# A fused attention and two-expert kernel: the first three chunks in a prologue of their own with a native fp32 first expert, and the slots left over made up two a step

## What is computed

```python
for t in range(S):
    cur = einsum('bhd,bhe->bhde', u[None] * kt, vt)
    y[:, :, t] = einsum('bhd,bhde->bhe', rt, state + cur)
    state = wt[:, :, :, None] * state + einsum('bhd,bhe->bhde', kt, vt)
x = y as 3072 tokens x 384
h = x @ w_in                      # 384 -> 1024
solu = h * softmax(h)
ln = (solu - mean) / sqrt(var + 1e-6) * g_ln
x2 = ln @ w_out                   # 1024 -> 384
h2 = x2 @ w_in2                   # 384 -> 2048
out = maximum(0.01 * h2, h2) @ w_out2   # 2048 -> 384
```

## Time and profile before

| | us |
|---|---|
| median of 3 runs (lowest, highest) | 835.58 (833.29, 835.66) |
| the profiled execution | 836.03 |
| its span, first to last instruction | 834.3 |
| TensorE busy in it | 787.2 |
| DVE / ACT / POOL busy in it | 538.0 / 320.0 / 215.6 |
| mean granted TensorE clock | 0.971 of full |

### The profile page before, as it was taken

The page is one execution under the profiler, slowest core; times in us unless marked ns, Lnnn a source line. Parts: engine busy times, 40 slices in busy tenths (PEclk is TensorE's granted clock), DMA queues, the critical chain, the costliest instruction groups (busy, mean ns, idle before and its releaser), DMA issues.

```text
span 834.3 us, 11926 instructions
## 1 busy us (share of the span) xinstructions
PE 787.2 (94%) x4570; PEld 746.7 (89%) x4570; DVE 538.0 (64%) x1116; ACT 320.0 (38%) x604; POOL 215.6 (26%) x224
## 2 busy tenths in 40 slices
PE   2866799999999999999999999999999999999996
PEld 1644689999999999999999999999999999999996
DVE  7777866666765775666766776657766676543332
ACT  2335433434432443334433443443433333334332
POOL 4667732123132132123122132123122222100000
PEclk9976599999999999999999999999999999999999
DMA  7772112113012032023022032023022030000000
GB/s 195 225 242 57 33 26 57 26 32 86 22 36 58 1 86 58 5 54 86 1 58 57 1 86 57 1 57 85 1 57 57 2 86 29 1 1 29 1 1 31
DMA packets 18844, 43.47 MB, mean 52 GB/s; under 512 B 2272, under 2 KB 14688, under 8 KB 18400
## 3 DMA queue, kind: packets, MB, share of 16 engines
q1 hardware_dynamic: 14736, 33.24, 16.5%
q10 hardware_dynamic: 4048, 9.44, 3.3%
HBM read 37.95 MB, written 4.72 MB: 51 GB/s over the span
## 4 chain that ended last, share of the span: by engine, by line
PE 86%; DVE 2%; ACT 1%; issue 0%; DVEq 0%; ACTq 0%
PE BANKS L961 59%; PE MISC L961 23%; PE BANKS L1072 2%; PE MISC L991 1%; PE MISC L984 1%; DVE state L768 0%; DVE att L722 0%; DVE RL L866 0%; ACT RH L629 0%; DVE Rraw L860 0%; DVE A L742 0%; ACT Rraw L622 0%; ACT W4H L556 0%; DVE ke L730 0%; ACT EXP L561 0%
## 5 line engine op out<-in xcount | busy, mean ns | idle before, releaser
L622 ACT ACTIVATE Rraw<-BANKS 128x384 f32<-128x384 f32 x128 | 62.9, 491 | 244.3 <-PE BANKS L961 244.2
L860 DVE TENSOR_TENSOR Rraw<-BANKS,Rraw 128x384 f32<-128x384 f32 x128 | 71.3, 557 | 124.5 <-ACT Rraw L622 124.0
L961 PE MATMUL BANKS<-RH,W4H 128*128 128x384 f32 x384 | 138.5, 361 | 0.9 <-DVE RL L866 0.8
L961 PE MATMUL BANKS<-X2H,W3H 128*128 128x384 f32 x384 | 130.4, 340 | 0.2 <-DVE X2L L872 0.2
L961 PE MATMUL BANKS<-X2L,W3H 128*128 128x384 f32 x384 | 129.2, 336 | 0.0
L961 PE MATMUL BANKS<-RH,W4L 128*128 128x384 f32 x384 | 129.0, 336 | 0.0
L961 PE MATMUL BANKS<-RL,W4H 128*128 128x384 f32 x384 | 129.0, 336 | 0.0
L961 PE MATMUL BANKS<-X2H,W3L 128*128 128x384 f32 x384 | 129.0, 336 | 0.0
L442 POOL TENSOR_TENSOR A<-ke,att 112x512 f32<-112x512 f32 x21 | 31.4, 1494 | 256.7 <-DVE att L734 256.7
L629 ACT ACTIVATE RH<-Rraw 128x384 fp32r<-128x384 f32 x128 | 67.1, 524 | 79.3 <-DVE Rraw L860 79.3
L730 DVE RECIPROCAL ke<-att 112x128 f32<-112x128 f32 x96 | 90.1, 941 | 0.0
(11 more groups left out here) (119 smaller groups left out, 1562.1 us busy)
## 6 DMA issues: line engine op xcount, KB each, us to landing
att<-rkw SPq DMA_DIRECT2D x48, 288.0 KB, 4.8
rtok<-r_tok SPq DMA_DIRECT2D x24, 192.0 KB, 5.0
ktok<-k_tok SPq DMA_DIRECT2D x24, 192.0 KB, 5.0
vtok<-v_tok SPq DMA_DIRECT2D x24, 192.0 KB, 5.1
out<-OUT SPq DMA_DIRECT2D x8, 576.0 KB, 6.0
W3raw<-w_in ACTq DMA_DIRECT2D x1, 3072.0 KB, 11.5
W4raw<-w_out ACTq DMA_DIRECT2D x1, 3072.0 KB, 24.7
W1raw<-w_in ACTq DMA_DIRECT2D x1, 1536.0 KB, 9.3
```

The lines of the kernel that those rows point to most:

```text
L622: nc.scalar.activation(Rraw[:, fp % 2, :], PR[fp % 2][:, 0:ST], ACT.Copy, scale=0.01).then_inc(act_slope, 1)
L860: nc.vector.tensor_tensor(Rraw[:, fp % 2, :], PR[fp % 2][:, 0:ST], Rraw[:, fp % 2, :], ALU.max).then_inc(dve_relu, 1)
L961: return nc.tensor.matmul(dst, lhsT, rhs, start=start, stop=stop, skip_group_check=True)
```

## The change

All engines get a prologue written out by hand for chunks 0 to 2 in place of `item` over 28 slots and the 8 M1 steps. In it:

- scores of a chunk go to two whole banks, are masked two pairs at a time (`first_mask`), and A holds all four pairs. Chunk 0's queries and keys go in halves (`portions`);
- the first expert is a plain fp32 product of x and the loaded W1 (`first_expert`), and the second product of expert one is plain fp32 of W2 and LN transposed and scaled by the gain, chunk by chunk (`first_out`, ACT's `take_ln`);
- ACT's queue loads all four weights at the start in the order W1, W3, W2, W4. W3 is split in the prologue (low parts on POOL), W1 and W2's low parts are made on POOL in the first M2 stage, W4's on DVE there; pieces are 768 columns;
- 24 slots are done when the M2 stage begins. In its first twelve steps two slots a step are run, the second behind `cons`; from the thirteenth on it is one, as before.

In all batches: the gain is no longer in W2 but a scale operand of the M1 copies on ACT and DVE; reciprocals have a tile of their own (ki), the range check sums ki and ct in two ACT passes in place of one POOL sum and one ACT pass; the decayed state is made on POOL (`decayed_state`), and DVE updates the state by two instructions of 192 columns in place of one of 384 and four of 96. The decay scans of the first chunks take their floor from PSUM.

```diff
+if opening and fp <= STEPS:
+    done = [min(CPS * SLOTS + 2 * j, F1 + LEAD + j) for j in (f, f + 1)]
+else:
+    done = [fp + LEAD - 1, fp + LEAD]
...
+def scores_of(m, a):
+    if m == 1:
+        return BANKS[:, (KM - 1 + a // 2) * 512:(KM + a // 2) * 512]
+    if m == 2:
+        return BANKS[:, a // 2 * 512:(a // 2 + 1) * 512]
+    return MISC[:, (a // 2 + 1) * 512:(a // 2 + 2) * 512]
...
+GROUPS = (4, 4, 8, 8)
...
+    def decayed_state(b, m):
+        wait(pool, dve_state, states(b, m - 1))
+        last = ct[:, m % 2, :, CH - 1:CH].broadcast_to([PD, PAIRS, PC])
+        nc.gpsimd.tensor_tensor(fresh[:, :, :], state[:, :, :], last, ALU.mult).then_inc(pool_decay, 1)
...
+    def low_part(w, g):
+        pool.wait_ge(split_hi[w], g + 1)
+        if w == 0:
+            pool.wait_ge(pe_h, 2 * CPS)
+        if w == 1:
+            pool.wait_ge(pe_cons, F1)
+        nc.gpsimd.tensor_tensor(group(los[w], w, g), group(raws[w], w, g),
...
+            if opening(b, kind, so):
+                if f < GROUPS[0]:
+                    low_part(0, f)
+                if F1 <= f < F1 + GROUPS[1]:
+                    low_part(1, f - F1)
...
+    own_token(0, 0, 0)
+    decayed_queries(0, 1)
+    own_token(0, 0, 1)
+    end_keys(0, 1)
+    decayed_state(0, 1)
+    own_token(0, 1, 0)
+    decayed_queries(0, 2)
+    for g in range(2):
+        low_part(2, g)
+    own_token(0, 1, 1)
+    end_keys(0, 2)
+    row_scale(0, 0)
+    decayed_state(0, 2)
+    own_token(0, 2, 0)
+    for g in range(2, 4):
+        low_part(2, g)
+    own_token(0, 2, 1)
+    decayed_queries(0, 3)
+    row_scale(0, 1)
+    end_keys(0, 3)
+    for g in range(4, 6):
+        low_part(2, g)
+    row_scale(0, 2)
+    for g in range(6, 8):
+        low_part(2, g)
...
+    def take_range(b, m):
+        wait(act, dve_inv, chunks(b, m, PAIRS, PAIRS))
+        for i, part in enumerate((ki[:, :, :], ct[:, m % 2, :, :])):
+            wait(act, act_range, chunks(b, m, 2, i))
+            nc.scalar.activation(junk[:, :, :], part, ACT.Copy,
+                                 accum_out=spread[:, bass.ds(chunks(b, m, 2, i), 1)]).then_inc(act_range, 1)
...
+        if attend and s == 7 and exists(b, m) and exists(b, m + 1):
+            take_range(b, m + 1)
...
+    def take_ln(m):
+        wait(act, pe_m1, m)
+        for f in range(F1):
+            wait(act, pe_lnT, m * 2 + f // 4 + 1)
+            nc.scalar.activation(first_ln[:, f, :], PR[f // 4][:, f % 4 * CH:(f % 4 + 1) * CH], ACT.Identity,
+                                 scale=gain[:, f:f + 1]).then_inc(act_lnT, 1)
...
+                if f % 2 == 0 and f // 2 + 2 < GROUPS[3]:
+                    high_part(3, f // 2 + 2)
+                if f % 2 == 1 and f // 2 < GROUPS[1]:
+                    high_part(1, f // 2)
...
+    for w in (0, 2, 1, 3):
+        load_weights(w)
+    take_range(0, 0)
+    take_keys(0, 0)
+    part_heads(0, 1)
+    take_x(0, 0)
+    take_range(0, 1)
+    for g in range(2):
+        high_part(2, g)
+    take_keys(0, 1)
+    exp_rows(0, 0)
+    part_heads(0, 2)
+    take_x(0, 1)
+    take_range(0, 2)
+    for g in range(2, 4):
+        high_part(2, g)
+    take_keys(0, 2)
+    normalise(0, 0)
+    exp_rows(0, 1)
+    take_x(0, 2)
+    for g in range(4, 8):
+        high_part(2, g)
+    normalise(0, 1)
+    part_heads(0, 3)
+    take_range(0, 3)
+    take_ln(0)
+    for g in range(2):
+        high_part(3, g)
+    take_ln(1)
+    exp_rows(0, 2)
+    for g in range(4):
+        high_part(0, g)
+    normalise(0, 2)
+    take_ln(2)
+    take_x2(0, 0)
...
+            wait(dve, pool_decay, fresh_count(b, m))
+            for h in range(2):
+                cols = slice(h * D, (h + 1) * D)
                 ins = nc.vector.scalar_tensor_tensor(
+                    state[:, :, cols], own[:, :, cols], heads[:, h * D:h * D + 1], fresh[:, :, cols],
                     ALU.mult, ALU.add)
...
+            for m, s in items[1:]:
+                item(b, m, s)
+                prepare(b, m, s, attend)
+                item_mid(b, m, s)
+                item_end(b, m, s)
+            if opening(b, kind, so) and f % 2 == 0:
+                low_part(3, f // 2)
...
+    decay(0, 1)
+    for a in (0, 2):
+        first_mask(0, a)
+    for a in range(PAIRS):
+        inverse(0, 1, a)
+    undecayed_keys(0, 1)
+    own_sums(0, 0)
+    take_y(0, 0)
+    take_state(0, 0)
+    for a in (0, 2):
+        first_mask(1, a)
+    decay(0, 2)
+    for a in (0, 1):
+        inverse(0, 2, a)
+    row_max(0, 0)
+    for a in (2, 3):
+        inverse(0, 2, a)
+    undecayed_keys(0, 2)
+    own_sums(0, 1)
+    take_y(0, 1)
+    take_state(0, 1)
+    times_exp(0, 0)
+    row_stats(0, 0)
+    row_moments(0, 0)
+    for a in (0, 2):
+        first_mask(2, a)
+    row_max(0, 1)
+    own_sums(0, 2)
+    take_y(0, 2)
+    take_state(0, 2)
+    times_exp(0, 1)
+    row_stats(0, 1)
+    row_moments(0, 1)
+    decay(0, 3)
+    for a in range(PAIRS):
+        inverse(0, 3, a)
+    undecayed_keys(0, 3)
+    row_max(0, 2)
+    times_exp(0, 2)
+    row_stats(0, 2)
+    row_moments(0, 2)
+    take_x2(0, 0)
...
+    def first_scores(m, pairs):
+        if m == 2:
+            pe.wait_ge(dve_he, 2)
+        for a in pairs:
+            ready = m * PAIRS + sum(n for at, n in portions(0, m) if at <= a)
+            pe.wait_ge(dve_keys, ready)
+            pe.wait_ge(act_rb, 2 * ready)
+            mm(scores_of(m, a)[:, a % 2 * 2 * CH:(a % 2 + 1) * 2 * CH], kt[:, m % 2, a, :],
+               rb[:, a, :, :].rearrange("p h t -> p (h t)"), a % 2 == 0, True).then_inc(pe_scores, 1)
...
+    def first_expert(m):
+        pe.wait_ge(act_x, m + 1)
+        if m == 0:
+            pe.wait_ge(ld_w[0], 16)
+        for n in range(FF1 // 512):
+            for k in range(KM):
+                last = mm(hidden(0, m)[:, n * 512:(n + 1) * 512], X[:, k, :], w1[:, k, n * 512:(n + 1) * 512],
+                          k == 0, k == KM - 1)
+            last.then_inc(pe_h, 1)
...
+    def first_out(m):
+        pe.wait_ge(act_ln, m + 1)
+        if m == 0:
+            pe.wait_ge(dve_he, 4)
+            pe.wait_ge(dve_decay, CPS * PAIRS)
+            pe.wait_ge(ld_w[1], 16)
+        for f in range(F1):
+            if m > 0 and f % 4 == 0:
+                pe.wait_ge(act_lnT, (m - 1) * F1 + f + 4)
+            last = nc.tensor.transpose(PR[f // 4][:, f % 4 * CH:(f % 4 + 1) * CH],
+                                       LN[:, m, f * 128:(f + 1) * 128], ident[:, :])
+            if f % 4 == 3:
+                last.then_inc(pe_lnT, 1)
+        for f in range(F1):
+            pe.wait_ge(act_lnT, m * F1 + f + 1)
+            for k in range(KM):
+                last = mm(ACC[k][:, m * CH:(m + 1) * CH], w2[:, f, k * 128:(k + 1) * 128], first_ln[:, f, :],
+                          m == 0 and f == 0, f == F1 - 1)
...
+    for m in range(CPS):
+        first_scores(m, range(PAIRS))
+        if m > 0:
+            first_expert(m - 1)
+        if m == 0:
+            first_attend(m, (0, 1))
+            first_keys(m)
+            first_attend(m, (2, 3))
+        else:
+            first_keys(m)
+            first_attend(m, range(PAIRS))
+        first_state(m)
+        first_transposes(m)
+    first_expert(CPS - 1)
+    for m in range(CPS):
+        first_out(m)
```

471 lines of the change are left out of this document (217 added, 254 removed).

## The result

The changed kernel takes 861.8 us (median; 860.34 to 862.96) against 835.62 of the kernel before on the same chip: 1.032 times as long, 95% interval 1.030 to 1.034. The prediction was 827.3 us with a range of 814 to 839. The profiled execution took 862.96 us with a span of 860.4, against 826.0 in my sum: 34.4 us too little.

What follows compares the result with a forecast made beforehand. Bound by a prologue with starved TensorE, then by TensorE itself. M2 start 96 + first M2 stage 86.7 + rest 643.3 = 826.0 us of span, so 827.3 us against the median of 835.58; range 814 to 839.

Steps and rivals of the forecast that it cites:

- What bounds the kernel: Whole kernel: a 126 us prologue with TensorE starved, then 708 us in which TensorE sets the pace.
- step (a): Prologue start: decay scan at 8.2 us, chunk 0's scores from 11.6 to 15.3, Pool's product at 21.9, dve_state at 23.0.
- (b): Prologue: chunk 0's expert done at 32.5 us; loads under the queued weights give chunk 2's scan at 32.2, tokens at 35.5.
- Step (c): Prologue: DVE's keys done at 39.0 us; Pool, after two W3 low parts, at the own-token product at 42.4; exponentials at 46.1.
- Step (f): End of prologue: chunk 0's output 5.2 us plus 1.8 for the low clock, to 77.9; M2 starts at 96, range 88 to 106.
- Rival 4: Prologue: native product not done or costing as the split one; time moves by 6 us at most; chance 0.02.
- the ten us for waits: Double steps: TensorE waits, 7 us over three chunks plus 3 for W1's last low part; bounds 2 and 20.
- rival 3: Double steps: Pool holds 21 DVE instructions; slower if the stage loses over 18.3 us, 854 us at 1.8 each; chance 0.14.
- The prediction's own sign of being wrong: First M2 product after 105 us, DVE's low parts in double steps averaging over 1 us, or a changed later part.
- 57 us of DVE in 61 of TensorE: Twelve double steps: DVE's summed work against TensorE's, in order, with waits for ACT between relu and low part.
- The 11.8 us for the twelve slots: First M2 stage: extra TensorE work for slots moved into it, making the stage 76.7 us without a new wait.
- What stays at nothing: Behind the first M2 stage: range sum, gain and Pool changes cost nothing, covered by consumption lagging two groups, 3 us and more.

Runs made afterwards that it cites:

- e1: Changed kernel with W4's load issued on ACT's queue only behind chunk 1's range sums: 857.16 us, 1.026 of the kernel before.
- e9: e8 with POOL making W3's first two low parts behind chunk 2's end keys, not ahead of chunk 1's second own-token product: 832.71 us, 0.996 of before.
- e3: Changed kernel with W1's high and low parts made in the prologue and POOL's W2 low parts only in steps 12 to 15: 849.96 us, 1.018 of before.
- e7: e1 and e3 together, with W2's four low parts made by DVE in the first M2 stage's last four steps: 841.85 us, 1.007 of before.
- e8: e7 with ACT's high parts and DVE's eight low parts of W4 made in the prologue: 836.32 us, 1.001 of before.
- e13: e9 with both range sums of a chunk moved from slot 7 of the chunk before to its own slot 1: 830.63 us, 0.995 of before.
- e12: e9 with the gain left out of the M1 copies on ACT and DVE: 831.36 us, 0.996 of before.
- e11: e9 with a chunk's first score waiting only for the half of the hidden rows it overwrites: 830.11 us, 0.994 of before.
- e5: e3 with unused POOL subtractions that read and write a free SBUF tensor, in eight double steps: 856.85 us, one run.

## Why the prediction was wrong, by its own steps

**What bounds the kernel** was right: what was won ahead of the steady part showed in the time, and TensorE's full part stayed full (610.87 of 620 us busy from 240 us on).

**Prologue, step (a), failed.** The four weight loads were put "queued from 8 us on", as if issuing cost ACT nothing. I looked at what the loads do to other loads and not at what queueing them does to the engine that issues. In the trace of before ACT issues at most two weights one behind the other (W3 at 34.18 in 0.37 us, W4 at 34.59 in 0.51), so no row showed it; the step had to be bounded and was not. e1: 9.1 us at the first score, 6.0 at M2, of the 8.0 by which M2 was missed. Given that, steps (a) and (b) hold to 0.6 us: first score 12.19 against 11.6, chunk 2's scan 32.16 against 32.2.

**Step (c) failed by about 1 us.** POOL's two low parts ahead of the own token were costed on POOL's queue, but not as a hold of DVE's keys: 2.64 us in the changed kernel, 4.47 in e1. The sum had POOL at the own-token product at 42.4; in e1 it is there at 43.34, behind a wait of 1.09 for DVE. Moving the parts gave 4.4 us (e9), but most of that is the queueing that the sum had priced. So e9's 95.21 beside the forecast 96 is no hit: e9 has an order that the forecast did not have, and e1, with the order forecast, has 97.94.

**Step (f)** held. The second product of the first expert, first the one behind a wait, then the next at full clock (24 products of two records each), in the changed kernel:

```profile
78.27 7.25 PE L1074 MATMUL BANKS<-OUT,W2raw 128*128 128x128 f32 x48 [4.53 <-ACT OUT L662]
...
86.47 5.62 PE L1074 MATMUL BANKS<-OUT,W2raw 128*128 128x128 f32 x48
```

5.62 / 24 = 0.234 us a product against an estimated 0.215, and 1.6 us more at the lower clock against 1.8; the 512-column product came at 5.42 / 6 = 0.90 against 0.86. Rival 4 had nothing in it.

**The double steps failed by 21.2 us**, in two terms. First, the ten us for waits left out what POOL's low parts do to DVE: e3 takes 18.65 us of the stage away by moving them. That includes W1's last part (5.13 us, where the sum had 3) and the low clock behind the waits, 7.1 us, for which the term had nothing. I had this as rival 3, with its trigger right (a stage loss over 18.3 us makes the change slower; it lost 31.2 over the clean stage) and its size wrong. I priced it at one POOL instruction for each of 21 DVE instructions, at most 1.8 us, and gave it 0.14 because the earlier trace rows showed 0.7. That 0.7 is a mean over four updates of which two were held. The maximum in the earlier trace rows, 2.42 us against a median of 0.31, is one of them, held for 2.1 us:

```profile
97.19 2.42 DVE L768 SCALAR_TENSOR_TENSOR state<-state,att,fresh 112x96 f32<-112x96 f32 x1
```

In the changed kernel two low parts were held, for 4.1 us each, through both of POOL's low parts; each was followed by a late mask with 3.7 us of TensorE idle. The update above and the one before it (1.29 us) were each held through one part of a gapless run, so the traces of before did not show that a hold can last for two. The prediction's own sign of being wrong, a mean over 1 us for the low parts in the double steps, came true with 1.26. The mean of 0.56 us in the earlier trace rows said nothing against it: it was taken over the whole kernel, nearly all of it without low parts on POOL. Second, the term "57 us of DVE in 61 of TensorE". DVE's side was near (54.3 in e7), TensorE's too small (67.7 recorded, 66.5 in e9). That both fit did not make it free: e8 takes W4's eight low parts, 8.0 us of DVE, and ACT's six high parts away and shortens the stage by 5.05. Without the low parts of W1, W2 and W4 on either engine beside the first twelve steps, the stage is 85.7 us, near my 86.7, but by other terms, so the nearness is luck: 3.9 us of idle time instead of 10, and 81.8 of work instead of 76.7. The 11.8 us for the twelve slots came to 16.9 (81.8 - 64.9), and what the 5.1 are is open.

**"What stays at nothing" failed** by 5.2 us, of which 4.5 lie behind the second M2 start. Mostly not for the reasons weighed there: the range sums cost nothing behind the stage (e13), the gain up to 1.8 us (e12), and the wait for both halves of the exponential's product, which I had not read out of the change, 3.3 (e11). The last two were measured each by itself and sum to more than the 4.5, so they overlap or are not that exact. The cover of "two groups, 3 us and more" covers what feeds a step's products; a chunk's score is not behind it, but in TensorE's own order.

**The chances** were off with that: rival 3 was the case that came, at 862 instead of 854, and "slower" had 0.15.

## What to carry to other kernels

A change that moves work to an idle engine has to be costed at the engines that share something with it: here eight long GpSimd instructions that read SBUF, 14.4 us of work, cost the stage 18.65 us where they stood beside VectorE. A mean over a few instructions hides such a hold; the longest one shows it. Where an engine both computes and issues large loads, look at what stands behind the issue in its own program, and issue only as many as were seen to go out fast. That an engine has time to spare in a stage does not make more work on it free there (e8). And each wait of TensorE should be compared old against new, line by line, before a later part is called unchanged.

## What the runs showed of the hardware

- The fourth weight load in a row on ACT's queue held ACT's sequencer for 11.04 us, while the three before it (W1, W3 and W2) took 0.38 to 0.51 each; issued 16 us later (e1) it took 0.42. The DMA engines, with SP's loads under way too, were busy for 0.87 of the first 20 us.
- A VectorE instruction with two inputs in SBUF waits for GpSimd instructions that read SBUF: 4.61, 4.59 and 4.84 us for one of 0.49 to 0.56, each through two low parts on POOL. It is not always held through a gapless run: beside two of POOL's own products it took 1.07, and in the kernel before each of two held updates waited for one part only. Beside e5's fillers, with a semaphore between them, it was 2.50; beside one of POOL's products and a memset, 1.08.
- TensorE's clock: behind an idle stretch of 4.53 us 24 products took 7.25 us, behind one of 3.17 us 5.62, as at full clock (e9, e13).
- A native fp32 product takes 0.234 us with 128 moving columns and 0.90 with 512, so here it goes by columns, and each leaves two records in the trace.
